# A new order of the opening on all engines: r and k sent ahead of v, a third score buffer, fewer dummy matmuls, tile 4 one step later

## What is computed

```python
def _attn_ref(r, k, v, w, u):                      # B, H, S, D = 4, 8, 768, 48
    for t in range(S):
        kt, vt, rt = k[:, :, t], v[:, :, t], r[:, :, t]
        cur = einsum('bhd,bhe->bhde', u[None] * kt, vt)
        y[:, :, t] = einsum('bhd,bhde->bhe', rt, state + cur)
        state = w[None, :, :, None] * state + einsum('bhd,bhe->bhde', kt, vt)
...
x = y as [3072 tokens, 384]
x = relu(x @ moe_w_in) ** 2 @ moe_w_out            # 384 -> 2048 -> 384
h = x @ moe2_w_in;  out = (h - tanh(h)) @ moe2_w_out
```

## Time and profile before

| | |
|---|---|
| median of 3 runs | 908.48 us (905.95 to 909.28) |
| profiled execution, its own time | 908.9 us |
| its span | 907.1 us |
| PE busy | 885.4 us, 98% of the span |
| DVE, POOL, ACT busy | 596.1, 489.4, 452.7 us |

### The profile page before, as it was taken

One profiled execution on the slowest core, in us unless ns is written; L12 is line 12 of the kernel. 1 busy time (PEld: TensorE's weight loads), 2 busy tenths in 40 slices (PEclk: granted clock), 3 DMA queues, 4 the chain that ended last, 5 costly groups with the idle time before them and its releaser, 6 DMA issues.

```text
span 907.1 us, 17344 instructions
## 1 busy us (share of the span) xinstructions
PE 885.4 (98%) x7048; PEld 733.5 (81%) x7048; DVE 596.1 (66%) x814; ACT 452.7 (50%) x858; POOL 489.4 (54%) x374
## 2 busy tenths in 40 slices
PE   8976999999999999999999999999999999999998
PEld 8765788888888888888888878888888888888886
DVE  5575664663665566454346668788787787787775
ACT  4433413322231332322123677777777777777775
POOL 7543443554354445243245777666666666666664
PEclk9987999999999999999999999999999999999999
DMA  5633111130311122030212000000000000000000
GB/s 213 203 105 132 58 58 58 58 115 1 114 58 58 58 92 81 5 110 3 104 36 104 35 1 1 35 1 1 35 1 0 35 1 1 36 0 1 36 1 35
DMA packets 11599, 47.18 MB, mean 52 GB/s; under 512 B 1408, under 2 KB 1536, under 8 KB 11520
## 3 DMA queue, kind: packets, MB, share of 16 engines
q1 hardware_dynamic: 11520, 46.08, 14.2%
HBM read 41.36 MB, written 4.72 MB: 51 GB/s over the span
## 4 chain that ended last, share of the span: by engine, by line
PE 90%; DVE 3%; ACT 2%; POOL 2%; DMA 1%; issue 1%; SPq 0%; ACTq 0%; DVEq 0%; POOLq 0%
PE acc L601 14%; PE acc L602 13%; PE acc L603 13%; PE hid L601 10%; PE hid L602 10%; PE hid L603 10%; PE sc L601 3%; PE sc L603 3%; PE sc L602 3%; PE y L664 2%; PE sc L635 2%; PE y L650 2%; DMA x2T<-in_nat 1%; PE y L608 1%; POOL wout_l L372 1%
## 5 line engine op out<-in xcount | busy, mean ns | idle before, releaser
L363 POOL TENSOR_TENSOR g_l<-g_f,g_h 128x512 fp32r<-128x512 f32 x96 | 129.4, 1348 | 198.3 <-ACT g_h L450 198.3
L601 PE MATMUL acc<-g_h,wout_h 128*128 128x512 f32 x564 | 223.9, 397 | 1.4 <-issue 0.8
L602 PE MATMUL acc<-g_l,wout_h 128*128 128x512 f32 x564 | 221.1, 392 | 0.0
L603 PE MATMUL acc<-g_h,wout_l 128*128 128x512 f32 x564 | 220.8, 392 | 0.0
L450 ACT ACTIVATE g_h<-g_f 128x512 fp32r<-128x512 f32 x96 | 60.5, 630 | 284.2 <-DVE g_f L890 283.6
L377 POOL TENSOR_TENSOR area<-area 128x512 f32<-128x512 f32 x96 | 125.9, 1312 | 103.9 <-ACT area L468 103.9
L601 PE MATMUL hid<-x_h,win_h 128*128 128x512 f32 x432 | 168.7, 390 | 0.5 <-DVE x_l L880 0.5
L602 PE MATMUL hid<-x_l,win_h 128*128 128x512 f32 x432 | 168.4, 390 | 0.0
L603 PE MATMUL hid<-x_h,win_l 128*128 128x512 f32 x432 | 168.1, 389 | 0.0
L382 POOL TENSOR_TENSOR g_l<-g_f,g_h 128x512 fp32r<-128x512 f32 x96 | 128.3, 1336 | 33.0 <-ACT g_h L483 33.0
L601 PEld LDWEIGHTS acc<-g_h,wout_h 128*128 128x128 f32 x564 | 106.6, 189 | 26.0 <-issue 1.7
(11 more groups left out here) (135 smaller groups left out, 1176.4 us busy)
## 6 DMA issues: line engine op xcount, KB each, us to landing
x2T<-in_nat SPq DMA_DIRECT2D x13, 736.0 KB, 6.0
area<-in_nat SPq DMA_DIRECT2D x11, 736.0 KB, 5.1
x2T<-in_tt SPq DMA_DIRECT2D x10, 512.0 KB, 3.8
area<-in_tt SPq DMA_DIRECT2D x10, 512.0 KB, 3.7
out<-x2T SPq DMA_DIRECT2D x18, 256.0 KB, 2.1
x2T<-in_win SPq DMA_DIRECT2D x4, 768.0 KB, 6.5
x2T<-in_wout SPq DMA_DIRECT2D x4, 768.0 KB, 8.2
area<-in_win SPq DMA_DIRECT2D x4, 768.0 KB, 4.3
```

The source lines that it names most:

```text
L363: pool.tensor_tensor(g_l[:, m % 4, :], g_f[:, m % 2, :], g_h[:, m % 4, :].bitcast(F32), ALU.subtract).then_inc(s_gl1, 1)
L601: pe.matmul(dst, wh, xh, start=first, stop=False)
L602: pe.matmul(dst, wh, xl, start=False, stop=False)
L603: return pe.matmul(dst, wl, xh, start=False, stop=last)
```

## The change

WARM_UP dummies grow from 6 to 7, and all later groups of dummies go (56 dummies). r and k of tiles 0 to 3 are loaded apart from and ahead of v, with semaphores of their own. A third score buffer lies in the memory of the state, so diagonal(2) waits for no attend, diagonal(3) only for attend(0) and diagonal(4) only for attend(3); the state is zeroed later, by one ACT copy of 128 x 1536 in place of a POOL memset. PE transposes and scores in another order. The first product, first1(0), is done in two halves of 256 tokens, the first of which needs tiles 0 and 1 only; POOL makes the low part of unit 0 in two pieces, after two of the decay_k. The low part of unit 1 moves from POOL to DVE, those of units 2, 5 and 7 from DVE to POOL. Tiles 4 to 7 get the slots at n = 2, 5, 8, 11 in place of 1, 4, 7, 10; score(4) and mask(4) move from step 0 to step 1. On SP, unit 2 moves behind the first three loads of tiles 4 and 5, and tile 6 ahead of unit 7.

```diff
-WARM_UP = 6
+WARM_UP = 7
...
          (state_all[:, b * PAIRS * 2 * D:(b + 1) * PAIRS * 2 * D] for b in range(B))]
-scores = [own.take(H * P).rearrange("p (g a t) -> p g a t", g=2, a=PAIRS) for _ in range(2)]
+scores = [x.rearrange("p (g a t) -> p g a t", g=2, a=PAIRS) for x in
+          (own.take(H * P), own.take(H * P), state_all[:, 0:H * P])]
...
+def scores_of(T):
+    return scores[2] if T == 2 else scores[0] if T == 3 else scores[T % 2]
 def decays(T):
     return 2 * (T + 1) if T < TPB else TPB + T + 1
 KV_FIRST = [0, 2, 1, 3]
+UPDATE_FIRST = [1, 3, 0, 2]
...
-LO_POOL = [[0, 1], [1, 3, 5, 7]]
+LO_POOL = [[0, 2, 5, 7], [1, 3, 5, 7]]
...
-    return TPB * (i + 1) + n // 3 if 0 <= i < BLOCKS - 1 and n % 3 == 1 and 0 <= n < 12 else None
+    return TPB * (i + 1) + n // 3 if 0 <= i < BLOCKS - 1 and n % 3 == (2 if i == 0 else 1) and 0 <= n < 12 else None
...
-SPLIT1_AT = {1: 3, 3: 4, 4: 5, 7: 6, 8: 7}
+HI1_AT = {3: 4, 4: 5, 6: 6, 7: 7}
+LO1_AT = {2: 3, 4: 4, 6: 5, 7: 6, 9: 7}
...
-        before = T - 2
-        if before < TPB:
-            sp.wait_ge(s_sc, before + 1)
-        else:
-            sp.wait_ge(s_y, before + 1)
+        sp.wait_ge(s_y, T - 1)
         load_tt(T)
-        if T < TPB + 2:
-            sp.wait_ge(s_kv, kv_count(T - TPB))
-        elif before < LAST_KV:
-            sp.wait_ge(s_kv, kv_count(before))
+        if T - 2 < LAST_KV:
+            sp.wait_ge(s_kv, kv_count(T - 2))
         load_nat(T)
     sp.dma_start(w_pow[:, 0, :], w_col).then_inc(s_w, 16)
-    load_nat(0)
+    load_rk(0)
     sp.dma_start(u_all, u_rep).then_inc(s_u, 16)
-    for T in range(1, TPB):
-        load_nat(T)
+    load_rk(1)
+    load_v(0)
+    load_rk(2)
+    load_v(1)
+    load_rk(3)
+    load_v(2)
+    load_v(3)
     load_unit1(0)
     load_unit1(1)
+    sp.wait_ge(s_sc, 3)
+    load_tt(TPB)
+    sp.wait_ge(s_sc, 4)
+    load_tt(TPB + 1)
+    sp.wait_ge(s_kv, kv_count(0))
+    load_nat(TPB)
     load_unit1(2)
-    load_tile(TPB)
-    load_tile(TPB + 1)
-    for n in range(3, UNITS):
-        load_unit1(n)
-    for T in range(6, TILES):
+    load_unit1(3)
+    sp.wait_ge(s_kv, kv_count(1))
+    load_nat(TPB + 1)
+    load_unit1(4)
+    load_unit1(5)
+    load_unit1(6)
+    load_tile(6)
+    load_unit1(7)
+    for T in range(7, TILES):
...
-    pool.wait_ge(s_u, 16)
+    def split_first():
+        hi, lo = unit_parts(0)
+        pool.wait_ge(*landed(0, 0))
+        pool.tensor_copy(hi, unit_raw(0, 0)).then_inc(s_whi0, 1)
+        pool.wait_ge(s_whi0, 1)
+        cut = 2 * P
+        pool.tensor_tensor(lo[:, :, 0:cut], unit_raw(0, 0)[:, :, 0:cut], hi[:, :, 0:cut].bitcast(F32),
+                           ALU.subtract).then_inc(s_lo0, 1)
+        pool.tensor_tensor(lo[:, :, cut:], unit_raw(0, 0)[:, :, cut:], hi[:, :, cut:].bitcast(F32),
+                           ALU.subtract).then_inc(s_wlo_p, 1)
     for T in range(TPB):
         products(T)
-    pool.wait_ge(*landed(0, 0))
-    pool.tensor_copy(unit_parts(0)[0], unit_raw(0, 0)).then_inc(s_whi0, 1)
-    split_lo(0, 0)
     pool.wait_ge(s_tab, 1)
     decay_k(KV_FIRST[0])
     decay_k(KV_FIRST[1])
+    split_first()
     decay_k(KV_FIRST[2])
     decay_k(KV_FIRST[3])
-    split_lo(0, 1)
     products(TPB)
+    split_lo(0, 2)
     for m in range(LAG):
         lo1(m)
+        if m == 1:
+            products(TPB + 1)
...
             T = prepare_at(i, n)
-            if T is not None:
+            if T is not None and T > TPB + 1:
                 products(T)
             if m + LAG < STEPS:
                 lo1(m + LAG)
+            if i == 0 and LO1_AT.get(n) in LO_POOL[0]:
+                split_lo(0, LO1_AT[n])
...
         act.wait_ge(s_c, T + 1)
-        after(act, s_y, T - 1)
+        if T >= 3:
+            act.wait_ge(s_y, {3: 1, 4: 4}.get(T, T - 1))
         for h in range(H):
             eye = ident[:, ::-1] if (h // 2) % 2 else ident
-            ins = act.activation(scores[T % 2][:, h % 2, h // 2, :], eye, ACT.Copy,
+            ins = act.activation(scores_of(T)[:, h % 2, h // 2, :], eye, ACT.Copy,
...
                        w_pow[rows, 7, :].unsqueeze(2).to_broadcast([D, PAIRS, D]), ACT.Copy).then_inc(s_tile, 1)
+    diagonal(0)
+    diagonal(1)
     act.wait_ge(s_powT, 1)
     act.activation(dec_k, acc2[:, :].rearrange("p (h e) -> p h e", h=H)[:, :, 0:D], ACT.Copy).then_inc(s_tab, 1)
-    diagonal(0)
-    diagonal(1)
     diagonal(2)
...
     x_high(2)
+    split_hi(0, 1)
     x_high(3)
-    split_hi(0, 1)
+    act.activation(state_all.rearrange("p (h t) -> p h t", t=P),
+                   ident.unsqueeze(1).to_broadcast([P, B * PAIRS * 2 * D // P, P]),
+                   ACT.Copy, scale=0.0).then_inc(s_stz, 1)
     split_hi(0, 2)
-    for m in range(LAG):
-        hi1(m)
+    hi1(0)
+    split_hi(0, 3)
+    hi1(1)
+    hi1(2)
...
-        dst, v, rT, sco, st = y_ps(T), v_of(T), rT_of(T), scores[T % 2], state[T % B]
+        dst, v, rT, sco, st = y_ps(T), v_of(T), rT_of(T), scores_of(T), state[T % B]
         opened = [False] * 4
         after(pe, s_xl, T - 1 if T < TPB else T)
         if T >= TPB:
-            pe.wait_ge(s_state, kv_count(T - TPB))
+            pe.wait_ge(s_state, max(TPB, T - TPB + 1))
...
-    def first1(m):
+    def first1(m, at=0, width=N):
         i, f = divmod(m, FT)
         after(pe, s_relu, m - 1)
         if f == 0:
-            pe.wait_ge(s_xl, TPB * (i + 1))
-        if f % Q == 0 and i == 0:
+            pe.wait_ge(s_xl, TPB * i + (at + width) // P)
+        if m < 2:
+            pe.wait_ge(s_lo0, 1)
+        elif m == 2:
+            pe.wait_ge(*lo_done(0, 0))
+        elif f % Q == 0 and i == 0:
             pe.wait_ge(*lo_done(0, 2 * (f // Q)))
+        ts = slice(at, at + width)
         for c in range(KC):
             fs = slice(P * f, P * f + P)
-            mm = product3(hid1[m % 2], win_h[:, c, fs], win_l[:, c, fs],
-                          x_h[:, i % 2, c, :], x_l[:, i % 2, c, :], c == 0, c == KC - 1)
-        mm.then_inc(s_h1, 1)
+            mm = product3(hid1[m % 2][:, ts], win_h[:, c, fs], win_l[:, c, fs],
+                          x_h[:, i % 2, c, ts], x_l[:, i % 2, c, ts], c == 0, c == KC - 1)
+        if at + width == N:
+            mm.then_inc(s_h1, 1)
...
         if m == 0:
-            pe.wait_ge(s_state, TPB)
+            pe.wait_ge(s_state, 2)
...
     transposed(0)
-    stay_warm(4, y7)
+    transposed(1)
+    pe.wait_ge(s_zero, 2)
+    score(0)
+    transposed(2)
+    score(1)
+    transposed(3)
     pe.wait_ge(s_pow, 4)
...
     mm.then_inc(s_powT, 1)
-    stay_warm(4, y7)
-    pe.wait_ge(s_zero, 2)
-    score(0)
-    transposed(1)
-    stay_warm(8, y7)
-    score(1)
-    transposed(2)
-    stay_warm(8, y7)
-    transposed(3)
-    stay_warm(8, y7)
     attend(0)
     score(2)
     pe.wait_ge(s_tab, 1)
-    stay_warm(8, acc2)
     attend(1)
     score(3)
-    stay_warm(8, hid34)
     attend(2)
-    stay_warm(8, hid34)
-    attend(3)
     key_value(KV_FIRST[0])
     key_value(KV_FIRST[1])
-    for m in range(LAG):
-        first1(m)
-        if m == 0:
-            key_value(KV_FIRST[2])
-            key_value(KV_FIRST[3])
+    attend(3)
+    first1(0, 0, N // 2)
+    first1(0, N // 2, N // 2)
+    first1(1)
+    first1(2)
+    key_value(KV_FIRST[2])
+    key_value(KV_FIRST[3])
...
             T = slot_at(i, n)
-            if m == 0:
+            if m == 1:
...
+    decay(3)
     bonus(3)
-    decay(3)
     mask(1)
     x_low(0)
     mask(2)
+    mask(3)
     x_low(1)
-    mask(3)
     x_low(2)
     x_low(3)
-    dve.wait_ge(s_const, 7)
-    update_state(KV_FIRST[0])
+    split_lo(0, 1)
     act1(0)
-    update_state(KV_FIRST[1])
-    update_state(KV_FIRST[2])
     act1(1)
-    update_state(KV_FIRST[3])
+    update_state(UPDATE_FIRST[0])
+    update_state(UPDATE_FIRST[1])
     act1(2)
-    split_lo(0, 2)
+    update_state(UPDATE_FIRST[2])
+    update_state(UPDATE_FIRST[3])
...
                 mask(T + 1)
+            if m == 1:
+                mask(TPB)
             if m + LAG < STEPS:
                 act1(m + LAG)
-            if m == 0:
-                mask(TPB)
             if T is not None:
...
                 bonus(T)
-            if i == 0 and SPLIT1_AT.get(n, 0) not in LO_POOL[0]:
-                split_lo(0, SPLIT1_AT[n])
+            if i == 0 and n in LO1_AT and LO1_AT[n] not in LO_POOL[0]:
+                split_lo(0, LO1_AT[n])
```

More of the change, by code:

```diff
@@ L118, in build @@
             "s_w", "s_u", "s_const", "s_setup", "s_pow", "s_powT", "s_tab", "s_tr", "s_tile", "s_whi0", "s_zero")
+        s_stz, s_lo0 = sems("s_stz", "s_lo0")
         s_tt = [sem(f"s_tt{i}") for i in range(2)]
         s_nat = [sem(f"s_nat{i}") for i in range(4)]
+        s_nat_rk = [sem(f"s_nat_rk{i}") for i in range(TPB)]
         s_dec, s_rk, s_ruk, s_kd, s_c, s_diag = sems("s_dec", "s_rk", "s_ruk", "s_kd", "s_c", "s_diag")
@@ L272, in load_nat, with load_rk, load_v @@
                 sp.dma_start(set_nat[set_of(T)], nat[T]).then_inc(s_nat[set_of(T)], 16)
+            def load_rk(T):
```

(29 more changed lines are left out.)

## The result

The changed kernel takes 892.85 us in the median of 4 runs (890.1 to 895.4) against 907.38 us for the kernel before in the same comparison: ratio 0.9833, 95% interval 0.9813 to 0.9853, a gain of 14.5 us. I had forecast 884.5 within 878 to 892, a gain of 24.1. The direction was right; the median lies 0.85 above my range. The profiled execution took 890.1, so against my sum (884.8) it misses by 5.3. One of the other three took 890.4, with the same mean granted clock of 0.998, and two took 895.3 and 895.4, with 0.994.

What follows compares the result with a forecast made beforehand. PE, nearly always busy, was taken as the bound, so pulling its work forward counts. Gain 12.3 + 19.0 - 7.0 - 0.2 = 24.1 us: 908.9 to 884.8 profiled, 884.5 for the median, range 878 to 892.

Steps and rivals of the forecast that it cites:

- The opening: Work before the first product: without the dummies first1(0) ends at 24.7 us instead of 37.04, gain 12.3.
- Rival C: Opening: PE stays at 1.2 GHz there, 7.7 us later, time 892; chance 0.12.
- The old holes: PE waits before score(4) and key_value(5), one of 0.8 and slow clock: 7.5 + 5.6 + 0.8 + 5.1 = 19.0 us.
- the 0.8 of "issue": One short PE wait of the kernel before, counted as 0.8 us within the 19.0 of the holes.
- the second hole: PE's 7.5 us wait before key_value(5) for mask(6); tile 6, loaded last, would land earlier and the wait go.
- the cure of the first: PE's 5.6 us wait before score(4) for decay(4): five us of PE work put between first1(2) and score(4).
- The waits after: New PE waits of the changed kernel: 2.0 + 0.85 + 0.3 + 3.8 = 7.0 us.
- second1(0) 2.0: New PE wait of 2.0 us at second1(0) for lo1(0) on POOL, behind unit 2, until 33.65.
- first1(8) 3.8: PE there at about 57, unit 4's low part on DVE ending at 61.0: wait 3.8 us.
- the lock of DVE and POOL: A DVE step beside a POOL step waits it out: a square took 1.75 us instead of 0.69.
- rival A: New waits larger: 3 us more of waits and one clock fall of 2.5, time 890; chance 0.22.
- two steps to spare: POOL's low parts of units 5 and 7, 3.52 us each in steps 6 and 9, each with two steps' slack.

Runs made afterwards that it cites:

- e4: Changed kernel with attend(3) ahead of the second key_value (tile 2) in PE's list: 893.4 us, ratio 0.9837.
- e7: Kernel before with the two loads of tile 6 ahead of unit 7 in SP's list, nothing else: 901.2 us, ratio 0.9926.
- e10: Changed kernel with tiles 4 to 7 back in their old slots, score(4) and mask(4) at step 0: 892.6 us, ratio 0.9836.
- e2: Changed kernel with 16 dummy matmuls on PE ahead of first1(8), filling its wait: 890.65 us, ratio 0.9811.
- a1: Changed kernel again, unedited, for a profile of a longer execution: 894.2 us, ratio 0.9852.
- e13: Changed kernel with DVE's low part of unit 6 moved behind mask(7): 893.9 us, ratio 0.9843.
- e6: Kernel before with the 56 dummy matmuls behind transposed(0) taken out, nothing else: 902.2 us, ratio 0.9939.
- e11: Changed kernel with 16 dummy matmuls ahead of first1(8) and 14 ahead of attend(6): 891.6 us, ratio 0.9824.
- e5: Changed kernel with unit 4's low part on POOL at step 2 and its high part one step earlier: 888.35 us, ratio 0.9785.
- e8: Changed kernel with unit 4's low part on POOL, and hi1(0), lo1(0) ahead of unit 2's high and low parts: 887.4 us, ratio 0.9769.
- e12: The kernel of e8 with 20 dummy matmuls ahead of attend(6): 887.0 us, ratio 0.9775.
- e14: The kernel of e8 with DVE's low part of unit 6 moved behind mask(7): 887.2 us, ratio 0.9770.

## Why the prediction was off

*The opening, 12.3 forecast.* Right in kind: first1(0) ends at 26.2 instead of 37.04, a gain of 10.8. The 1.5 that are missing are the stop before attend(3). Behind it x_high(3) and x_low(3) come late: DVE waited 2.86 and ended x_low(3) at 24.98, where I had the second half of first1(0) start at 23.7. e4 shows that the stop is not attend(3)'s own, but stands at a place in PE's instruction stream. It cost nothing further on: second1(0) waits for unit 2 in any case, and its wait got shorter by what PE came later. Rival C did not happen: transposes and halves ran at the upper level from 5 us on. That was in part luck: I had taken decay(0) at 6.88, as behind transposes at the lower level, and it started at 6.08.

*The old holes, 19.0 forecast.* Right: both gone, with their clock falls. But the 0.8 of "issue" in that sum is not theirs, and a stop of 0.8 stands in the changed kernel too. e7 shows that the second hole was for the most part the place of tile 6 in SP's list: worth 6.4 us alone in the median. The move of tiles 4 to 7 by one step, which I took for the cure of the first, is worth nothing by itself (e10): the wait of 6.6 before score(4) goes, and the waits before first1(8) and at key_value(6) grow from 2.2 and none to 3.6 and 1.6.

**The waits after, 7.0 forecast: this is the step that failed.** Its parts: second1(0) 2.0, measured 0.97; score(4) 0.85, measured 0.8; 0.3 for mask(5), measured none; first1(8) 3.8, measured 3.6. Those were drawn rightly, with the lock of DVE and POOL in them, but the close figure at first1(8) is luck: it starts at 62.4 where I had 61.0, and PE was there at 58.9 where I had 57. The 1.4 are not the late opening carried along. relu(2) started 0.9 late (34.58), since unit 2 landed at 28.10 and not 27.3, and the rows of tile 6, which I had landed near 52 and hidden, landed at 54.35 and kept DVE waiting for 0.92. What was left out: the clock fall behind first1(8), 1.7 us (e2 wins 2.0), which I had priced only in rival A; and the wait of key_value(6) for mask(7), 1.6 to 2.7, with a fall of 1.7 of its own in a1. I had written that POOL's low part of unit 5 has two steps to spare. It has, but it locks out DVE's step meanwhile, and I drew those meetings only up to 61 us. e13 shows that mask(7) was late for the step ahead of it, and that the DVE list has no slack to hide that step; the same order with POOL's step moved away was not run.

*The sum for the profiled execution.* In the terms of the forecast: 1.5 (opening) + 0.8 ("issue", still there) + 1.7 (clock) + 1.6 (key_value(6)) + 0.6 (one more wait for g_l at 102), less 1.7 by which the waits of the list were shorter (5.3 of 7.0), is 4.5 of a miss of 5.3 (884.8 against 890.1). Of the other 0.8, 0.25 is a second such stop at 48.05; the rest stays open. The median lies 2.7 higher still; the one longer execution that was profiled (a1) had a longer first fall, a larger wait at key_value(6) and a fall there. This is near rival A, "3 us of more waits and one fall", 890, at 0.22; it should have been the forecast, since a wait of 3.8 in my own sum stood close to one behind which the clock had fallen.

*What stays open.* Of the parts of the change only the dummies (e6, 5.4) and the place of tile 6 (e7, 6.4) were run alone and the slots undone (e10); r and k ahead of v, the third score buffer, the two halves of first1(0) and the moved low parts were not, so how they share the rest of the 14.5 is not shown. e11 shows 3 us of spread with the clock up; unequal stops for "issue" and unequal landings of unit 2 were seen in single profiles (e11, e5), but how the spread divides between them was not measured. The kernels e8, e12 and e14 are equal within their intervals, 887.0 to 887.4, about 2.3% under the kernel before and 0.6% under the changed one.

## What to carry to other kernels

When a step is called hidden because its result is due later, look also at which other engine it shuts out while it runs, and who stands behind that. When a wait of PE is left in a forecast, price a fall of the clock with it. Moving a step within a full engine's list only pays if its next due time has slack; the slots (e10) and unit 6 (e13, e14) both gave back what they won within one to five steps. A stop that isn't in the chain to the next hole can be shortened and bring nothing, as in e4: follow the chain first.
